# Interleaving the attention of token thirds 2 and 3 with the layers, and a regrouped seven-product scheme with results kept in four PSUM banks

## The chip, the cores and the metric

The kernel runs on one core of a Trainium2 chip. The metric is the device time of one execution in microseconds (us); the median of repeated executions counts. A profile of one execution gives the engines' timelines: TensorE (PE, with its weight loads PEld), VectorE (DVE), ScalarE (ACT), GpSimd (POOL) and the queue of SyncE (SP) that issues the transfers.

## What is computed

Windowed attention, then a gated layer, then a second gated layer whose last two matrices stand one behind the other. All is fp32.

```python
# q, k, v: (4, 8, 576, 64); window 128; ALiBi slopes by head
scores = q @ k.T / sqrt(64) + bias            # masked to 0 <= rel < 128
attn = softmax(scores) @ v
x = attn.transpose(0, 2, 1, 3).reshape(2304, 512)
x = (sigmoid(x @ w_gate) * (x @ w_val)) @ w_out          # d_ff 1536
out = ((x @ w1) * (x @ w2)) @ w3 @ w_out2                # d_ff 1024
```

## The kernel before

Every fp32 operand of a product is split into two fp32r parts, hi (a rounded copy, made on ACT) and lo (the rest, a subtraction on DVE or POOL). One product is then three matmuls: hi*hi, hi*lo, lo*hi (function `product`, lines 424 to 426).

**Attention stage.** 16 pairs (batch, two heads) of 5 steps give 80 steps, NSTEP. A software pipeline of 90 slots (SLOTS) runs them, each engine with its own order written out by hand and with lags between the parts: `scores` on PE (for both heads at once, q laid out in blocks on the diagonal over 128 partitions, for up to two query blocks of 64, 256 key columns each), `score` on DVE (bias and row minimum), `exponentials` on ACT, `reciprocals` on DVE, `normalise` on POOL, `turn` on PE (up to four transposes), `turned_hi` on ACT, `turned_lo` on DVE, `pv` on PE, `out_copy` on ACT. Into the same slots go the splits of q, k and v, and 64 products `fold(k)`, which multiply w3 by the last matrix once, so that the second layer needs one matrix less. The activations xf of all 2304 tokens are complete before the layers begin.

**Layer stage.** Tokens go in three passes (NPASS) of 768. In a pass, 6 groups (G1) of 256 hidden columns of layer 1 and 4 groups (G2) of layer 2 follow each other, 30 groups in all. A group has two halves, gate (m=0) and value (m=1). Each half is one 2x2 block multiplication done with seven products of the Strassen kind, `multiply(g, m, ...)`, 42 matmuls of 384 columns, into three banks quad_ps; ACT copies two of them out (`keep_21`, `keep_12`), DVE forms the four results in SBUF (`combine`), ACT applies the gate (Sigmoid in layer 1, Copy in layer 2), DVE multiplies and splits. `project(g)` then makes 8 output tiles of 6 matmuls in three banks o_ps, which DVE adds into xf (`add_up`, 551 ns each). PE runs `project(g-1)` behind the halves of g; after the last group of a layer (`last_of`) its own projection follows at once, and the next layer, an "instance", can start only from its sums: five sums of x blocks on DVE and POOL (`x_sum`), seven hi copies on ACT (`xs_hi_part`), seven lo parts (`x_lo_part`). The order of the products is M2, M4, M5, M3, M1, M7, M6. POOL forms five sums of weight blocks for each half (`weight_sum`) and their lo parts (`weights_lo`). SP loads one half's weights (512 KB) when the ones before have been split.

Of the kernel before, what the change touches and what calls it, by code (L numbers as in the profile page):

```python
# [7 lines left out]
ALU = mybir.AluOpType  # L8
# [4 lines left out]
P = 128  # L13
B, H, S, D = 4, 8, 576, 64
WINDOW = 128
# [3 lines left out]
QB = 64  # L19
NQ = S // QB  # L20
KW = WINDOW + QB
HP = H // 2
PAIRS = B * HP
STEPS = (NQ + 1) // 2
NSTEP = PAIRS * STEPS
VC = (S + P - 1) // P
# [11 lines left out]
NQUAD = 2 * NG  # L38
SCALE = 1.0 / D ** 0.5
MASKED = -1e9  # L40
RAWS = 4


M2, M4, M5, M3, M1, M7, M6 = range(7)

W_S5, W_S2, W_D6, W_D7, W_S1, W_11, W_22 = range(7)
W_OF = {M2: W_S2, M4: W_22, M5: W_S5, M3: W_11, M1: W_S1, M7: W_D7, M6: W_D6}

BANK_OF = {M2: 0, M4: 1, M5: 2, M3: 0, M1: 2, M7: 1, M6: 2}

C11, C12, C21, C22 = 0, 1, 2, 3

HI_IN = {r + 2: r for r in range(IB)}
LO_IN = {r + 3: r for r in range(IB)}

LAG_QK, LAG_SCORE, LAG_NORM, LAG_TURN, LAG_PV, LAG_OUT = 4, 5, 6, 7, 9, 9
LAG_FOLD = 6
NFOLD = IB * IB
SLOTS = NSTEP + LAG_OUT + 1

X_SUM_SLOT = {M4: 48, M3: 54, M1: 60, M7: 66, M6: 72}
X_HI_SLOT = {M2: 48, M4: 49, M5: 52, M3: 55, M1: 61, M7: 67, M6: 73}
X_LO_SLOT = {M2: 50, M4: 51, M5: 53, M3: 57, M1: 63, M7: 68, M6: 75}
W_SUM_SLOT = {71: (0, 0), 72: (0, 1), 73: (0, 2), 77: (1, 0), 78: (1, 1), 79: (1, 2)}
W_HI_SLOT = {74: 0, 80: 1}
W_LO_SLOT = {75: 0, 81: 1}

RAW_SLOT = 66
# [22 lines left out]

def build(nc, qT, kT, v, bias8, ident, w3t, wo2, w_gate, w_val, w_out, w1, w2, outT):
    scratch = nc.dram_tensor("w3_times_wout", (IB, P, DM), F32, kind="Internal").ap()
    ctx = ExitStack()
    with ctx:
        def sb(scope, name, shape, dt):
            return scope.enter_context(nc.sbuf_tensor(name, shape, dt))

        def sem(name):
            return ctx.enter_context(nc.semaphore(name))  # L100

        xf = sb(ctx, "xf", [P, KB * T], F32)
        xs_hi = sb(ctx, "xs_hi", [P, 7 * 2 * TH], F32R)
        xs_lo = sb(ctx, "xs_lo", [P, 7 * 2 * TH], F32R)
        xsum = [sb(ctx, "xsum0", [P, 2 * TH], F32)]

        with ExitStack() as one:
            wo2_raw = sb(one, "wo2_raw", [P, RAWS * DM], F32)
            w3_raw = sb(one, "w3_raw", [P, IB * P], F32)
            w3_hi = sb(one, "w3_hi", [P, IB * P], F32R)  # L110
            w3_lo = sb(one, "w3_lo", [P, IB * P], F32R)
            wo2_hi = sb(one, "wo2_hi", [P, IB * DM], F32R)
            wo2_lo = sb(one, "wo2_lo", [P, IB * DM], F32R)
            q_raw = sb(one, "q_raw", [P, S], F32)
            k_raw = sb(one, "k_raw", [P, S], F32)
            v_raw = sb(one, "v_raw", [P, VC * P], F32)
            q_hi = [sb(one, f"q_hi{b}", [P, NQ * P], F32R) for b in range(2)]
            q_lo = [sb(one, f"q_lo{b}", [P, NQ * P], F32R) for b in range(2)]
            k_hi = [sb(one, f"k_hi{b}", [P, S], F32R) for b in range(2)]
            k_lo = [sb(one, f"k_lo{b}", [P, S], F32R) for b in range(2)]  # L120
            v_hi = [sb(one, f"v_hi{b}", [P, VC * P], F32R) for b in range(2)]
            v_lo = [sb(one, f"v_lo{b}", [P, VC * P], F32R) for b in range(2)]
            bias = sb(one, "bias", [P, HP * KW], F32)
            eye = sb(one, "eye", [P, P], F32)
            negs = [sb(one, f"negs{b}", [P, 2 * KW], F32) for b in range(2)]
            exps = [sb(one, f"exps{b}", [P, 2 * KW], F32) for b in range(2)]
            prob = [sb(one, f"prob{b}", [P, 2 * (2 * P + QB)], F32) for b in range(2)]
            pt_hi = [sb(one, f"pt_hi{b}", [P, 4 * P], F32R) for b in range(2)]
            pt_lo = [sb(one, f"pt_lo{b}", [P, 4 * P], F32R) for b in range(2)]
            negmax = sb(one, "negmax", [P, 4], F32)  # L130
            rowsum = sb(one, "rowsum", [P, 4], F32)
            rowsum2 = sb(one, "rowsum2", [P, 4], F32)
            recip = sb(one, "recip", [P, 4], F32)
            fold_sb = sb(one, "fold_sb", [P, DM], F32)

            pA = [one.enter_context(nc.psum_tensor(f"score_ps{b}", [P, 512], F32)) for b in range(2)]
            fold_ps = [one.enter_context(nc.psum_tensor(f"fold_ps{b}", [P, 512], F32)) for b in range(2)]
            pB = [one.enter_context(nc.psum_tensor(f"turn_ps{b}", [P, 512], F32)) for b in range(2)]
            pC = [one.enter_context(nc.psum_tensor(f"pv_ps{b}", [P, 512], F32)) for b in range(2)]

        raw_q = [sb(ctx, f"raw_q{m}", [P, PIECE], F32) for m in range(2)]
        raw_o = sb(ctx, "raw_o", [P, PIECE], F32)
        wsum = [sb(ctx, f"wsum{m}", [P, 5 * GW], F32) for m in range(2)]
# [3 lines left out]
        wo_hi = [sb(ctx, f"wo_hi{b}", [P, PIECE], F32R) for b in range(2)]  # L147
        wo_lo = [sb(ctx, f"wo_lo{b}", [P, PIECE], F32R) for b in range(2)]
        side = sb(ctx, "side", [P, 4 * TH], F32)
        hid = sb(ctx, "hid", [P, 4 * TH], F32)  # L150
        h_hi = [sb(ctx, f"h_hi{b}", [P, 4 * TH], F32R) for b in range(2)]
        h_lo = [sb(ctx, f"h_lo{b}", [P, 4 * TH], F32R) for b in range(2)]
        s21 = sb(ctx, "s21", [P, TH], F32)
        s12 = sb(ctx, "s12", [P, TH], F32)
        u11 = sb(ctx, "u11", [P, TH], F32)
        t22 = sb(ctx, "t22", [P, TH], F32)
        xsum += [sb(ctx, f"xsum{k}", [P, 2 * TH], F32) for k in range(1, 5)]

        qc = ctx.enter_context(nc.psum_tensor("quad_ps2", [P, 512], F32))
        gate_ps = [ctx.enter_context(nc.psum_tensor("gate_ps0", [P, 512], F32))]  # L160
        qa, qb = [ctx.enter_context(nc.psum_tensor(f"quad_ps{k}", [P, 512], F32)) for k in (0, 1)]
        quad_ps = [qa, qb, qc]
        gate_ps.append(ctx.enter_context(nc.psum_tensor("gate_ps1", [P, 512], F32)))
        ps_o = [ctx.enter_context(nc.psum_tensor(f"o_ps{o}", [P, 512], F32)) for o in range(3)]

        q_in, k_in, v_in = sem("q_in"), sem("k_in"), sem("v_in")
        bias_in, eye_in = sem("bias_in"), sem("eye_in")
        w3_in = [sem("w3_in0"), sem("w3_in1")]
        wo2_in = [sem(f"wo2_in{r}") for r in range(RAWS)]
        small_zeroed = sem("small_zeroed")  # L170
        zeroed = [sem("zeroed_q0"), sem("zeroed_rest")]
        q_hi_done, q_split = sem("q_hi_done"), [sem("q_split0"), sem("q_split1")]
        k_hi_done, k_split = sem("k_hi_done"), sem("k_split")
        v_hi_done, v_split = sem("v_hi_done"), sem("v_split")
        w3_hi_done, w3_split = sem("w3_hi_done"), sem("w3_split")
# [7 lines left out]
        rawq_in, rawo_in = [sem("rawq_in0"), sem("rawq_in1")], sem("rawo_in")  # L183
        wsum_done = [sem("wsum_done0"), sem("wsum_done1")]
        wq_hi_done = [sem("wq_hi_done0"), sem("wq_hi_done1")]
        wq_split = [sem("wq_split0"), sem("wq_split1")]
        wo_hi_done, wo_split = sem("wo_hi_done"), sem("wo_split")
        xsum_done = [sem(f"xsum_done{j}") for j in range(7)]
# [3 lines left out]
        s21_done, s12_done, u11_done = sem("s21_done"), sem("s12_done"), sem("u11_done")  # L192
        t22_done = sem("t22_done")
        c_done = [sem(f"c{k}_done") for k in ("11", "12", "21", "22")]
# [4 lines left out]
        def where(n):  # L199

            return n // STEPS, n % STEPS

        def blocks_of(i):

            return (0, 1) if 2 * i + 1 < NQ else (0,)

        def chunks_of(i):

            return (1,) if i == 0 else (0, 1)

        def seen(i, j):

            return max(0, 2 - (2 * i + j)) * QB

        def two(ap):

            return ap[:, :].rearrange("p (j c) -> p j c", j=2)[:, :, 0:KW]

        def diagonal(x, h):

            return x[h * D:(h + 1) * D, :].rearrange("p (j h c) -> p j h c", h=2, c=QB)[:, :, h, :]

        def blocks(x, h):

            return x[h * D:(h + 1) * D, :].rearrange("p (j c) -> p j c", c=QB)

        def raw_block(r):
            return wo2_raw[:, (r % RAWS) * DM:(r % RAWS + 1) * DM]

        def turned_cols(i):  # L230

            lo, n = chunks_of(i)[0], len(blocks_of(i))
            return lambda ap: ap[:, :].rearrange("p (c n) -> p c n", c=2)[:, lo:2, 0:n * P]

# [915 lines left out]
```

## Time and profile before

| | us |
|---|---|
| median of 3 runs | 971.6 (970.73 to 973.06) |
| the profiled execution's own time | 972.31 |
| its span, first to last instruction | 970.5 |
| PE busy | 899.5 |
| POOL busy | 722.3 |
| DVE busy | 689.1 |
| ACT busy | 505.8 |
| mean granted clock of TensorE | 0.979 |

The span is what the profiler saw of the execution; 1.8 us lie around it. Busy time counts an instruction from its start to its modelled end, and matmuls in a row overlap: a matmul that is recorded with 0.33 us starts 0.17 us behind the one before it. For PE, the distance from start to start is the price, not the recorded duration.

### The profile page before, as it was taken

The numbers are of one execution on the slowest core, as the hardware profiler recorded it, in microseconds if no ns is written. First come the engines' busy times: TensorE is split into PE (matmuls) and PEld (weight loads), VectorE is DVE, ScalarE is ACT, GpSimd is POOL, SyncE is SP. The second block draws the span as 40 slices with busy tenths as digits, with TensorE's granted clock in tenths as the row PEclk, the third lists the DMA queues.
The fourth block names the chain that finished last, engine by engine and source line by source line (L and its number), as shares of the span: only waits on it lengthen the run. The fifth ranks groups of instructions, "written<-read, shape, count | busy, mean of one in ns | idle before, by whom it ended". The sixth has DMA issues, their size and how long they took to land.

```text
span 970.5 us, 15723 instructions
## 1 busy us (share of the span) xinstructions
PE 899.5 (93%) x5272; PEld 869.0 (90%) x5272; DVE 689.1 (71%) x1506; ACT 505.8 (52%) x1139; POOL 722.3 (74%) x535
## 2 busy tenths in 40 slices
PE   3999989868999997999999999799999999989998
PEld 3889877767899997899889999789988999988998
DVE  7988899885666668577756666857785666686666
ACT  4888878767544443544454444354444444435441
POOL 6778877876887775998679777489867977738940
PEclk9999999979999999999999999999999999998999
DMA  7333432410222210222142222012113211211301
GB/s 235 105 108 113 121 95 78 143 47 23 86 76 78 66 66 22 72 82 69 41 140 79 66 83 71 22 66 87 66 44 131 87 66 66 67 42 52 102 1 66
DMA packets 37409, 75.92 MB, mean 78 GB/s; under 512 B 3153, under 2 KB 16081, under 8 KB 37329
## 3 DMA queue, kind: packets, MB, share of 16 engines
q1 hardware_dynamic: 37328, 74.92, 23.9%
q8 instruction: 42, 0.69, 0.3%
q14 instruction: 39, 0.31, 0.1%
HBM read 68.09 MB, written 6.82 MB: 77 GB/s over the span
## 4 chain that ended last, share of the span: by engine, by line
PE 71%; DVE 14%; ACT 7%; issue 5%; POOL 2%; DMA 1%; SPq 0%; ACTq 0%; DVEq 0%; POOLq 0%
PE quad_ps L424 15%; PE quad_ps L426 14%; PE quad_ps L425 14%; PE o_ps L424 8%; PE o_ps L426 8%; PE o_ps L425 8%; DVE rowsum L766 3%; DVE xs_lo L811 2%; ACT exps L584 2%; DVE negs L755 1%; DVE xf L879 1%; POOL prob L1007 1%; ACT pt_hi L595 1%; DVE pt_lo L775 1%; ACT wq_hi L630 1%
## 5 line engine op out<-in xcount | busy, mean ns | idle before, releaser
L424 PE MATMUL quad_ps<-xs_hi,wq_hi 128*128 128x384 f32 x840 | 286.9, 342 | 25.4 <-ACT s L646 22.0
L426 PE MATMUL quad_ps<-xs_hi,wq_lo 128*128 128x384 f32 x840 | 284.6, 339 | 0.0
L425 PE MATMUL quad_ps<-xs_lo,wq_hi 128*128 128x384 f32 x840 | 284.5, 339 | 0.0
L424 PEld LDWEIGHTS quad_ps<-xs_hi,wq_hi 128*128 128x128 f32 x840 | 160.8, 191 | 31.7 <-issue 16.5
L1041 POOL TENSOR_TENSOR wq_lo<-wsum,wq_hi 128x1280 fp32r<-128x1280 f32 x60 | 177.3, 2955 | 9.4 <-ACT wq_hi L630 9.4
L424 PE MATMUL o_ps<-h_hi,wo_hi 128*128 128x384 f32 x480 | 161.2, 336 | 3.2 <-DVE xf L879 3.1
L425 PEld LDWEIGHTS quad_ps<-xs_lo,wq_hi 128*128 128x128 f32 x840 | 160.7, 191 | 0.0
L426 PEld LDWEIGHTS quad_ps<-xs_hi,wq_lo 128*128 128x128 f32 x840 | 160.5, 191 | 0.0
L426 PE MATMUL o_ps<-h_hi,wo_lo 128*128 128x384 f32 x480 | 160.4, 334 | 0.0
L425 PE MATMUL o_ps<-h_lo,wo_hi 128*128 128x384 f32 x480 | 160.4, 334 | 0.0
L1037 POOL TENSOR_TENSOR wq_lo<-raw_q,wq_hi 128x512 fp32r<-128x512 f32 x60 | 77.7, 1295 | 105.8 <-ACT wq_hi L624 105.8
L879 DVE TENSOR_TENSOR xf<-o_ps,xf 128x384 f32<-128x384 f32 x192 | 103.5, 551 | 43.6 <-PE o_ps L426 43.6
L661 ACT ACTIVATE gate_ps<-side 128x384 f32<-128x384 f32 x120 | 59.6, 498 | 76.4 <-DVE h_lo L867 55.4
L424 PEld LDWEIGHTS o_ps<-h_hi,wo_hi 128*128 128x128 f32 x480 | 90.1, 188 | 5.8 <-DVE xf L879 5.8
L646 ACT COPY s<-quad_ps 128x384 f32<-128x384 f32 x60 | 28.7, 479 | 120.2 <-PE quad_ps L426 120.1
L425 PEld LDWEIGHTS o_ps<-h_lo,wo_hi 128*128 128x128 f32 x480 | 90.1, 188 | 0.0
L426 PEld LDWEIGHTS o_ps<-h_hi,wo_lo 128*128 128x128 f32 x480 | 90.1, 188 | 0.0
L668 ACT CAST h_hi<-gate_ps 128x384 fp32r<-128x384 f32 x120 | 57.6, 480 | 59.6 <-DVE gate_ps L862 59.6
L1047 POOL TENSOR_TENSOR wo_lo<-raw_o,wo_hi 128x1024 fp32r<-128x1024 f32 x30 | 72.0, 2401 | 17.9 <-ACT wo_hi L638 17.9
L584 ACT ACTIVATE exps<-negs,negmax 128x192 f32<-128x192 f32 (+1 forms) x144 | 62.0, 432 | 42.9 <-DVE negmax L755 40.9
L867 DVE TENSOR_TENSOR h_lo<-gate_ps,h_hi 128x384 fp32r<-128x384 f32 x120 | 65.9, 549 | 23.8 <-ACT h_hi L668 23.3
L1062 POOL TENSOR_TENSOR wsum<-raw_q 128x512 f32<-128x512 f32 x60 | 81.8, 1363 | 0.0
(89 smaller groups left out, 1893.8 us busy)
## 6 DMA issues: line engine op xcount, KB each, us to landing
raw_q<-w SPq DMA_DIRECT2D x24, 512.0 KB, 3.5
raw_q<-w_gate SPq DMA_DIRECT2D x18, 512.0 KB, 3.5
raw_q<-w_val SPq DMA_DIRECT2D x18, 512.0 KB, 3.5
raw_o<-w_out SPq DMA_DIRECT2D x18, 512.0 KB, 3.5
raw_o<-w_times_wout SPq DMA_DIRECT2D x12, 512.0 KB, 3.6
k_raw<-kT SPq DMA_DIRECT2D x16, 288.0 KB, 2.9
q_raw<-qT SPq DMA_DIRECT2D x16, 288.0 KB, 3.0
v_raw<-v SPq DMA_DIRECT2D x16, 256.0 KB, 2.7
```

The lines of the kernel that those rows point to most:

```text
L424: pe.matmul(out, lh, rh, start=start, stop=False, skip_group_check=onto)
L425: pe.matmul(out, lh, rl, start=False, stop=False, skip_group_check=onto)
L426: return pe.matmul(out, ll, rh, start=False, stop=stop, skip_group_check=onto)
L584: op = nc.scalar.activation(exps[buf][:, cols], negs[buf][:, cols], ACT.Exp, scale=-1.0, bias=negmax[:, 2 * buf + j:2 * buf + j + 1], accu ...
L661: nc.scalar.activation(gate_ps[n % 2][:, 0:TH], side[:, piece(k)], func).then_inc(gated, 1)
L668: nc.scalar.copy(h_hi[g % 2][:, piece(k)], gate_ps[n % 2][:, 0:TH]).then_inc(h_hi_done, 1)
L867: nc.vector.tensor_tensor(out=h_lo[g % 2][:, piece(k)], in0=gate_ps[n % 2][:, 0:TH], in1=h_hi[g % 2][:, piece(k)], op=ALU.subtract).then_i ...
L879: op = nc.vector.tensor_tensor(out=xf[:, cols], in0=ps_o[t % 3][:, 0:TH], in1=xf[:, cols], op=ALU.add)
L1037: nc.gpsimd.tensor_tensor(out=wq_lo[m][:, cols].rearrange("p (b n) -> p b n", b=2), in0=four[:, 0:4:3, :], in1=wq_hi[m][:, cols].rearrange ...
L1041: nc.gpsimd.tensor_tensor(out=wq_lo[m][:, 0:5 * GW], in0=wsum[m][:, :], in1=wq_hi[m][:, 0:5 * GW], op=ALU.subtract).then_inc(wq_split[m], 1)
L1047: nc.gpsimd.tensor_tensor(out=wo_lo[g % 2][:, :], in0=raw_o[:, :], in1=wo_hi[g % 2][:, :], op=ALU.subtract).then_inc(wo_split, 1)
L1062: op = nc.gpsimd.tensor_tensor(out=out[:, 2 * GW:4 * GW], in0=raw[:, 0:2 * GW], in1=raw[:, 2 * GW:4 * GW], op=ALU.subtract)
```

## The change

The number of attention steps stays 80, but they are cut by token third: a job is (third, pair of heads, batch, first query, steps), a step has 128 queries of two heads. The first third (28 steps) runs ahead of the layers, in 36 slots together with all 64 folds, two to a slot; the 24 steps of the second third run inside pass 0 of the layers, and the 28 of the third inside pass 1, one in each "section" (a half or a projection; 30 sections in a pass). Scores are multiplied for each head by itself, 64 contraction rows, into a bank of each head. The small addition to the row sum moves from DVE to ACT. The layers use another form of the seven products: four operand sums in place of five for x and for the weights, products P2 and P4 accumulated onto P1 and P7 in PSUM, the results left in their four banks, where gate, product and split read them. One bank copy a half on ACT (`keep`) and five additions on DVE stand in place of two copies and six additions. The projection has two banks in place of three, since two banks are now attention's. xf holds two thirds of the tokens' columns in place of three.

```diff
+PARTS = (((0, 0, 3), (0, 384, 2), (1, 0, 2)), ((1, 192, 3), (2, 0, 3)), ((2, 384, 2), (3, 0, 3), (3, 384, 2)))
+JOBS = [(third, hp, b, q0, n) for third in range(NPASS) for hp in range(HP) for b, q0, n in PARTS[third]]
...
-BANK_OF = {M2: 0, M4: 1, M5: 2, M3: 0, M1: 2, M7: 1, M6: 2}
+BANK_OF = {P1: 0, P2: 0, P6: 1, P3: 1, P5: 2, P7: 3, P4: 3}
+BANK_OUT = {C11: 0, C12: 1, C22: 2, C21: 3}
...
-LAG_QK, LAG_SCORE, LAG_NORM, LAG_TURN, LAG_PV, LAG_OUT = 4, 5, 6, 7, 9, 9
+LAG_QK, LAG_SCORE, LAG_NORM, LAG_TURN, LAG_PV = 3, 4, 5, 6, 8
+SLOTS = HEAD + LAG_PV
...
+def fold_slot(k):
+
+    return 5 + k // 2
...
+        quad = [ps(f"quad_ps{k}") for k in range(4)]
+        ps_o = [ps(f"o_ps{k}") for k in range(2)]
+        attn = [ps(f"attn_ps{k}") for k in range(2)]
...
+            sp.wait_ge(zeroed, 1)
+            load_k(0)
...
+                sides = ((q_hi, k_hi), (q_hi, k_lo), (q_lo, k_hi))
+                for t, (left, right) in enumerate(sides):
+                    for h in range(2):
+                        rows = slice(h * D, (h + 1) * D)
+                        mm = pe.matmul(score_bank(n, h)[:, keys], left[st][rows, q], right[st][rows, where],
+                                       start=t == 0, stop=t == 2)
+                mm.then_inc(qk_done, 1)
...
+            for sec, (g, kind, of) in enumerate(SECTIONS):
+                n, m = step_at(sec), step_at(sec - 1)
+                if n is not None:
+                    scores(n)
+                if kind == "proj":
+                    for k in range(8):
+                        project(of, k)
+                        if k == 1 and m is not None:
+                            turn(m)
+                        if k == 5 and m is not None:
+                            pv(m)
+                else:
+                    for j in range(7):
+                        multiply(2 * g + (kind == "val"), j)
+                        if j == P5 and m is not None:
+                            turn(m)
+                        if j == P7 and m is not None:
+                            pv(m)
...
+            def keep(q):
+
+                act.wait_ge(prod_done, product_done(q, P1))
+                wait(act, u2_done, q)
+                nc.scalar.copy(s1[:, :], quad[0][:, 0:TH]).then_inc(s1_done, 1)
...
+            def sums_26(q):
+
+                dve.wait_ge(prod_done, product_done(q, P6))
+                dve.wait_ge(s1_done, q + 1)
+                wait(dve, c_done[C21], q)
+                nc.vector.tensor_tensor(out=u2[:, :], in0=quad[1][:, 0:TH], in1=s1[:, :], op=ALU.add
+                                        ).then_inc(u2_done, 1)
+                dve.wait_ge(u2_done, q + 1)
+                wait(dve, c_done[C12], q)
+                nc.vector.tensor_tensor(out=u25[:, :], in0=quad[2][:, 0:TH], in1=u2[:, :], op=ALU.add
+                                        ).then_inc(u25_done, 1)
...
+                elif kind == "val":
+                    sums_26(2 * g + 1)
+                    if m is not None:
+                        turned_lo(m)
+                    if n is not None:
+                        reciprocals(n)
+                    hidden(g, C11)
+                    result_22(2 * g + 1)
+                    hidden_lo(g, C11)
+                    hidden(g, C22)
+                    result_12(2 * g + 1)
+                    hidden(g, C12)
+                    hidden_lo(g, C22)
+                    result_21(2 * g + 1)
...
+                elif g % GP == G1 - 1:
+                    for k in range(3):
+                        add_up(of, k)
+                    if m is not None:
+                        turned_lo(m)
+                    if n is not None:
+                        reciprocals(n)
+                    add_up(of, 3)
+                    x_sum(inst, P5)
+                    add_up(of, 4)
+                    add_up(of, 5)
+                    x_sum(inst, P6)
+                    x_lo(inst, P5)
```

The products of a half run in the order P1, P5, P6, P2, P7, P3, P4; P2 waits for `keep`, P3 for the sum u2, P4 for result C22 in its bank. The first product into each bank waits for the gate (on a value half) or for the lo split (on a gate half) that reads the bank last.

## Rows read from the trace of the kernel before

**Rows 1.** The page: span, and the share of each engine's busy time.
```profile
span 970.5 us, 15723 instructions
PE 899.5 (93%) x5272; PEld 869.0 (90%) x5272; DVE 689.1 (71%) x1506; ACT 505.8 (52%) x1139; POOL 722.3 (74%) x535
```
**Rows 2.** Busy time by stretch: PE, PEld, DVE, ACT, POOL, clock, DMA.
```profile
60.00:90.00 30.00, 29.14 (x206) 26.14 (x204) 26.74 (x97) 25.24 (x88) 24.03 (x28) 1.00 0.40 114
...
238.00:968.00 730.00, 700.98 (x3947) 691.82 (x3946) 490.48 (x885) 323.52 (x544) 539.79 (x332) 0.98 0.20 68
...
256.00:370.00 114.00, 114.00 (x656) 113.68 (x657) 72.16 (x142) 49.17 (x84) 88.35 (x56) 1.00 0.22 74
...
370.00:403.00 33.00, 26.51 (x141) 25.58 (x140) 26.09 (x37) 16.63 (x26) 22.62 (x14) 0.95 0.10 34
469.00:508.00 39.00, 35.20 (x187) 33.27 (x186) 24.90 (x41) 15.48 (x27) 27.76 (x18) 0.96 0.28 94
```
**Rows 3.** PE in order of time, layer stage: start, us; 65 starts apart.
```profile
405.58 0.33 PE L425 MATMUL quad_ps<-xs_lo,wq_hi 128*128 128x384 f32 x1
...
416.85 0.33 PE L424 MATMUL o_ps<-h_hi,wo_hi 128*128 128x384 f32 x1
```
**Rows 4.** PE in order of time where an instance begins.
```profile
384.17 0.45 PE L424 MATMUL quad_ps<-xs_hi,wq_hi 128*128 128x384 f32 x1 [4.95 <-ACT s L646]
384.42 0.52 PE L425 MATMUL quad_ps<-xs_lo,wq_hi 128*128 128x384 f32 x1
...
387.89 0.34 PE L424 MATMUL quad_ps<-xs_hi,wq_hi 128*128 128x384 f32 x1
```
**Rows 5.** Who waited for whom: total us, times, longest.
```profile
PE quad_ps L424 <- ACT s L646: 22.0, 8, 4.9
```
**Rows 6.** PE in order of time, one attention slot and its fold.
```profile
63.30 0.28 PE L425 MATMUL score_ps<-k_lo,q_hi 128*128 128x256 f32 x1
...
63.89 0.28 PE L424 MATMUL pv_ps<-pt_hi,v_hi 128*128 128x256 f32 x1
...
64.26 0.60 PE L455 MATMUL turn_ps<-eye,prob 128*128 128x128 f32 x4
64.61 0.48 PE L424 MATMUL fold_ps<-wo_hi,w_hi 128*128 128x512 f32 x1
...
65.16 0.40 PE L426 MATMUL fold_ps<-wo_hi,w_lo 128*128 128x512 f32 x1
```
**Rows 7.** Groups by line and shape: busy us, mean ns, idle before.
```profile
L1041 POOL TENSOR_TENSOR wq_lo<-wsum,wq_hi 128x1280 fp32r<-128x1280 f32 x60 | 177.3, 2955 | 9.4 <-ACT wq_hi L630 9.4
L1047 POOL TENSOR_TENSOR wo_lo<-raw_o,wo_hi 128x1024 fp32r<-128x1024 f32 x30 | 72.0, 2401 | 17.9 <-ACT wo_hi L638 17.9
L1065 POOL TENSOR_TENSOR wsum<-raw_q 128x256 f32<-128x256 f32 x60 | 48.7, 812 | 0.0
L584 ACT ACTIVATE exps<-negs,negmax 128x192 f32<-128x192 f32 x112 | 50.3, 450 | 37.0 <-DVE negmax L755 36.3
L755 DVE CUSTOM_DVE_ANT_0 negs<-score_ps,bias 128x192 f32<-128x192 f32 x112 | 34.9, 343 | 0.0
L775 DVE TENSOR_TENSOR pt_lo<-turn_ps,pt_hi 128x512 fp32r<-128x512 f32 x48 | 33.0, 688 | 3.9 <-ACT pt_hi L595 3.6
```
**Rows 8.** ACT in order of time at the first Sigmoid.
```profile
239.69 0.48 ACT L652 COPY s<-quad_ps 128x384 f32<-128x384 f32 x1
240.19 1.28 ACT L661 ACT_TABLE_LOAD   x1
241.49 0.49 ACT L661 ACTIVATE gate_ps<-side 128x384 f32<-128x384 f32 x1
```
**Rows 9.** Start and end: first load, first fold, last addition.
```profile
0.73 0.39 SPq L313 DMA_DIRECT2D k_raw<-kT  x1
...
17.00 0.63 PE L424 MATMUL fold_ps<-wo_hi,w_hi 128*128 128x512 f32 x1
...
967.65 0.56 DVE xf L879
```

More of the change, by code:

```diff
@@ L119, in build @@
[L119 to L126, printed above, removed]
@@ L1025, in x_lo_part, with x_sum @@
-            def x_lo_part(inst, j):
+                cols = heads(soft[buf])[0:rows, :, keys]
+                nc.gpsimd.tensor_tensor(
+                    out=cols, in0=cols,
+                    in1=recip[0:rows, 2 * buf:2 * buf + 2].unsqueeze(2).to_broadcast([rows, 2, keys.stop - keys.start]),
+                    op=ALU.mult).then_inc(norm_done, 1)
+            def x_sum(inst):
+                wait_x(pool, inst, P7)
+                wait(pool, xs_split[P7], inst)
+                nc.gpsimd.tensor_tensor(out=pair_of(xt[2][:, :]), in0=b_block(inst, 1, 1), in1=b_block(inst, 0, 1),
+                                        op=ALU.subtract).then_inc(t_done[P7], 1)
@@ new lines, in _ @@
+                if s == 30:
+                    plain_lo(0, 0)
+                    sums_lo(0, 0)
+                if s == 32:
+                    weight_sums(0, 1)
+                if s == 34:
+                    plain_lo(0, 1)
+            x_sum(0)
+            for j in (P7, P3, P4):
+                x_lo(0, j)
+            for sec, (g, kind, of) in enumerate(SECTIONS):
+                n = step_at(sec)
+                more, inst = g + 1 < NG, instance(g) + 1
+                if kind == "gate":
+                    sums_lo(g, 1)
+                    if more:
+                        weight_sums(g + 1, 0)
+                elif kind == "val":
+                    out_lo(g)
+                    if more:
+                        weight_sums(g + 1, 1)
+                elif of == g - 1 and more:
+                    plain_lo(g + 1, 0)
+                    sums_lo(g + 1, 0)
+                if n is not None:
+                    normalise(n)
+                splits(sec)
+                if kind == "val" and first_of(g):
+                    plain_lo(g + 1, 0)
+                    sums_lo(g + 1, 0)
+                    plain_lo(g + 1, 1)
+                if kind == "proj" and of == g - 1 and more:
+                    plain_lo(g + 1, 1)
+                    if g % GP == GP - 1:
+                        x_lo(inst, P1)
+                if kind == "proj" and of == g and more:
+                    if g % GP == G1 - 1:
+                        x_lo(inst, P1)
+                    x_sum(inst)
+                    for j in (P7, P3, P4):
+                        x_lo(inst, j)
```

1497 lines of the change are left out of this document (775 added, 722 removed).

## The prediction

> **What bounds the kernel now.** The page comes first: PE is busy for 93% of the span, POOL for 74% [rows 1]. A mean over stages says little, so I read busy time by stretch next [rows 2]. In the attention stretch from 60 to 90 us PE has 29.1 of 30 us, DVE 26.7, ACT 25.2, POOL 24.0: all four are close to full, and none of them can be relieved alone. In the steady layer stretch from 256 to 370 us PE has all of it, POOL 78%, DVE 63%, ACT 43%. So the layers have free time on three engines, and attention has none on any. The third view is PE in order of time. In steady layers 65 starts lie within 11.27 us, 0.1733 us for a matmul of 384 columns [rows 3]. From 238 to 968 us there are 3947 matmuls, 684 us at that rate out of 730 [rows 2]: 46 us are lost. The losses sit where an instance begins: from 370 to 403 us 141 matmuls (24.4 us of work) take 33 us, 8.6 us lost, three times in the kernel; from 469 to 508 us 187 (32.4) take 39, 6.6 us lost, twice. PE there waited 4.95 us for the first bank copy, itself late behind seven x splits, and then ran for some 3.5 us at half the rate, 0.315 us a matmul, so at the lower level of its clock, 1.2 GHz [rows 4]. Such waits sum to 22.0 us over the kernel [rows 5].
>
> The time before is, in these terms: 235 us until the layers alone hold PE (two products are already among the last attention steps), 3960 x 0.1733 = 686 us, 46 us lost and 3 us behind the last matmul (the last addition starts at 967.65 [rows 9]). That is 970 us, and the execution has 1.8 us around its span, 972.3; the median is 0.7 us lower.
>
> **The head: what is left ahead of the layers.** A full attention step costs PE: six score matmuls (63.30 to 63.89 is five of them, 0.12 each) 0.71 us, six of pv 0.73, four transposes 0.35 (64.26 to 64.61) [rows 6]: 1.8 us. The start of a batch saves about 0.9 of it (128 keys, one chunk); 8 of the first 28 steps are such. A fold is three matmuls of 512 columns, two starts in 0.55 us and a third near 0.22, some 0.73 us [rows 6]; two in a slot make 1.45. Mean slot on PE: 1.8 - 0.26 + 1.45 = 3.0 us. DVE: score twice, 343 ns at 192 columns [rows 7], so about 0.93 at 256 with the reads of the minimum, the lo part 0.69, the reciprocal 0.17, and the splits of v and w3 and the copies of the fold about 1.0: 2.8. POOL: normalise about 1.1, k, q and v lo 1.3, w3 0.4: 2.8. ACT 2.5. In the stretch of rows 2 PE kept 97% with DVE at 89%, so a slot takes 3.1 us. The first fold stands at 17.0 us [rows 9]. The change holds SP back until DVE has cleared six tiles (about 2.4 us), with the first load at 0.73 before, but it asks for fewer bytes by the first step and waits for no buffer: 19 us. Then 28 slots x 3.1 = 87, three slots with little in them 5, and the last eight folds 5.8, which cover the x sums of POOL and DVE. **Head: 117 us** (bounds 108 and 130: all slots at PE's 3.0 with the old start, and 3.5).
>
> **The layers.** Products and projections keep their number: 3960 x 0.1733 = **686 us**. The 52 moved steps now cost PE time that nothing covers: 52 x 1.8 - 8 x 0.9 = **86 us**. This is the price of the move; 118 us of head go against it.
>
> **Losses at instances.** The form with four sums needs x only by tiles: P1 wants two output tiles, P5 four, and the first bank copy stands ahead of nothing that is late. I follow the end of layer 1: with the last tile done at T, P1 starts at T, P5 at T+1, P6 waits for x_sum, hi and lo on DVE until T+3.2 (1.1 late), P4 0.7 late. With no long pause there is nothing that lowers the clock. 2 us three times, 1 us twice; the second group, which follows with no projection between, waits for lo splits of the value half, 1.5 us six times: **17 us** in place of 46 (bounds 8 and 46).
>
> **Losses inside sections.** Here the trace of before shows nothing like it. The short loop is turn, hi on ACT, lo on DVE, pv: about 1.6 us with handovers, against three products of 1.04 us between turn and pv, but DVE has to make u2 and u25 first, and these wait for P6: the lo part is ready 3.05 us after the turn, pv comes at 3.12. The other orders have 1 us or more to spare: P4 waits for C22 with pv and P3 between. So most sections fit and some miss by tenths; I take 0.3 us, 52 x 0.3 = **16 us** (bounds 0, and 1.5 us a step, a late engine in each section, near the longest DVE piece between two duties). Per group of 28 us POOL has: eight block sums of 812 ns, 6.5; lo of 768 and 1024 columns for two halves, about 8.5 (between 812 ns at 256 and 2955 at 1280); wo_lo 2.4 [rows 7]; normalise 2.6 to 3.0; q, k, v lo 2.9 to 4.9. That is 23 to 25 us, under PE, with slack of a section between each product of POOL and its use. DVE has 26 operations of about 0.5 us and 5 us of attention, 19; DMA is at a fifth [rows 2]. DVE's last value operation runs 1.6 us into the projection, which the two banks just bear.
>
> **The table of ACT.** Exp and Sigmoid did not share a table: at the first Sigmoid a load of 1.28 us stands, and the activation begins 0.02 us behind it [rows 8]. In passes 0 and 1 the 12 groups of layer 1 alternate twice each, 24 loads, 31 us of ACT. ACT then has about 21 of 28 us in such a group, and the gate it delays is wanted 2 us later: nothing on the path. It costs 0.5 us each if the value half's lo part falls behind it, which is in my upper bound.
> The Trainium skill (ScalarE: Activation LUTs, "What ACT_TABLE_LOAD costs") adds a drain of about 1.38 us to each switch, 64 us of ACT in place of 31; the row shows no such gap. By the page ACT would be near 24 of 28 us, and the sum for PE would move to its upper bound.
>
> **Sum.** 117 + 686 + 86 + 17 + 16 + 3 = 925 us of span, 926.8 with what lies around it, some 0.7 less as a median: **926 us**, 4.7% below 971.6. A measurement of this kernel can tell 0.2%, 2 us, from no change.
>
> **Rivals.**
> *The two heads overlap on PE.* Each head's scores use 64 rows and a bank of their own, interleaved. If pairs run together, six matmuls cost three: 0.35 us less, 52 times in the layers, 18 us, and nothing in the head, where DVE and POOL are as full: 908 us. No row here has a matmul of 64 rows, so the trace speaks neither way.
> The Trainium skill states such overlap (TensorEngine Tiling (Array Packing), "Theoretical Speedup", up to 2x) and that a change of tiling mode drains PE ("Key Properties"); two drains a step would give back part of the gain, and no row shows either.
> *The losses at instances stay.* If x splits still gate the first half (POOL's lo part of 768 columns lasts about 2 us), the 17 us go back to 46: 955 us. Against it: P1 and P5 no longer wait for seven splits.
> *A late lo part in each section.* At 0.8 us a step, 26 us more: 952 us.
> *Slower than before.* One mechanism: the fixed orders of DVE and ACT chain turn, lo and pv behind a product's sums each time, and PE stands in all 52 steps. It decides at 0.3 + 45/52 = 1.2 us a step. At 1.5 us: 926 + 62 = 988 us. For it: DVE's margin in the loop is under 0.1 us and table loads lengthen ACT's part. Against it: one miss can't be longer than the operation ahead.
>
> **Chances.** Forecast, 915 to 940 us: 0.50. Heads overlap, 898 to 915: 0.20. Instances or lo parts, 940 to 962: 0.16. Slower: 0.10. Else, under 898 or near 971: 0.04. Range 898 to 962 leaves 0.14 out. Faster by over 0.2%: 0.87; within: 0.02; slower: 0.11.
>
> **What would show it.** In the changed kernel's PE timeline: the first product of the layers near 117 us; score matmuls at 0.12 us from start to start (0.06 for the overlap); no pause over 2 us at instance starts and no stretch at 0.32 us a matmul; waits of pv for the lo part under 0.3 us in the mean; 25 table loads or so on ACT. A head over 130 us, or waits of PE for DVE beyond 30 us in sum, would make it wrong.

## The result, and the profile after

The changed kernel takes 1018.9 us (median of 4 runs, 1016.8 to 1020.5), the kernel before 972.0 beside it: ratio 1.0482 (1.0457 to 1.0506), 4.8% slower. The forecast was 926, its range 898 to 962. Both its size and its sign were wrong. Two of the experiments below, e10 and e12, had one execution each that was far slower than its fellows (4918 and 1744 us); it is left out of their times.

The page of the changed kernel, answering to [rows 1]:

```profile
span 1017.9 us, 16149 instructions
PE 919.8 (90%) x5352; PEld 855.0 (84%) x5352; DVE 602.1 (59%) x1364; ACT 549.9 (54%) x1259; POOL 737.3 (72%) x626
```

Busy time by stretch (the stretch, its length, then PE, PEld, DVE, ACT, POOL, clock, DMA share, GB/s). First the head in three stretches, then the six stretches in which an instance begins, then the whole layer stage; the second block has the five between the starts:

```profile
19.00:60.00 41.00, 37.79 (x226) 28.13 (x224) 25.38 (x86) 25.99 (x93) 25.91 (x29) 1.00 0.34 107
60.00:110.00 50.00, 44.34 (x272) 33.51 (x269) 31.55 (x104) 34.13 (x122) 35.69 (x42) 0.97 0.43 137
110.00:134.00 24.00, 18.63 (x95) 14.60 (x94) 14.39 (x28) 13.14 (x35) 21.30 (x21) 0.93 0.12 39
134.00:168.00 34.00, 27.84 (x158) 26.00 (x157) 17.68 (x41) 22.95 (x46) 32.50 (x26) 0.90 0.38 132
310.00:352.00 42.00, 30.70 (x173) 28.73 (x172) 26.55 (x48) 22.19 (x48) 37.30 (x25) 0.88 0.12 39
425.00:470.00 45.00, 33.24 (x179) 30.76 (x178) 24.69 (x50) 21.47 (x42) 33.52 (x27) 0.90 0.27 90
620.00:662.00 42.00, 30.08 (x166) 27.94 (x165) 26.74 (x48) 21.33 (x48) 33.83 (x26) 0.88 0.13 42
745.00:780.00 35.00, 24.70 (x125) 23.24 (x124) 17.11 (x23) 12.21 (x18) 23.59 (x17) 0.90 0.25 91
900.00:945.00 45.00, 35.83 (x183) 34.28 (x182) 27.03 (x38) 18.28 (x29) 34.86 (x26) 0.92 0.18 60
134.00:1015.00 881.00, 816.10 (x4754) 776.47 (x4752) 521.84 (x1125) 467.53 (x990) 647.49 (x525) 0.97 0.22 72
```
```profile
168.00:310.00 142.00, 140.50 (x866) 131.85 (x865) 86.27 (x217) 94.08 (x215) 105.74 (x89) 1.00 0.25 81
352.00:425.00 73.00, 72.91 (x437) 70.82 (x436) 44.37 (x97) 37.83 (x79) 55.20 (x47) 1.00 0.19 63
470.00:620.00 150.00, 148.69 (x906) 138.93 (x905) 86.97 (x222) 99.73 (x235) 112.06 (x103) 1.00 0.26 84
662.00:745.00 83.00, 82.56 (x506) 77.82 (x505) 49.29 (x121) 48.05 (x121) 63.18 (x58) 1.00 0.19 64
780.00:900.00 120.00, 119.78 (x682) 117.92 (x681) 72.97 (x142) 49.07 (x81) 86.47 (x67) 1.00 0.21 71
```

In the five stretches between, PE has 564.4 of 568 us at a granted clock of 1.00. The steady sections run as they were meant to, with the moved steps inside. The six stretches of the starts last 243 us, hold 984 starts of PE, and the clock there is 0.88 to 0.92. If every one of them were a full matmul of 384 columns at 0.1733 us, they would fill 171 us, so at least 72 us are lost there (attention's matmuls are shorter). POOL is the busiest engine in four of the six (37.3 of 42 us, 32.5 of 34).

Against the sum, whose head and layer stage were 117 and 805 us: the layers begin at 134 (the head is 17 us too long), and the layer stage lasts 881, which is 686 + 86 + 109 of losses where 33 were forecast.

One start is that from pass 0 to pass 1. Its chain, in three views in order of time (start, duration), is SP's queue, then ACT, then PE:

```profile
440.90 0.40 SPq L501 DMA_DIRECT2D outT<-xf  x1
441.34 0.50 SPq L479 DMA_DIRECT2D raw_q<-w_gate  x1
441.89 1.02 SPq L488 DMA_DIRECT2D wo_lo_raw<-w_out  x1
```
```profile
450.03 1.04 ACT L818 CAST wo_hi<-wo_lo_raw 128x1024 fp32r<-128x1024 f32 x1 [6.61 <-DMA wo_lo_raw<-w_out]
451.09 1.28 ACT L837 ACT_TABLE_LOAD   x1
452.38 0.49 ACT L837 ACTIVATE sig<-quad_ps 128x384 f32<-128x384 f32 x1
```
```profile
453.02 0.66 PE L576 MATMUL quad_ps<-xs_hi,wq_hi 128*128 128x384 f32 x1 [4.65 <-ACT sig L837]
...
454.11 0.52 PE L576 MATMUL quad_ps<-xs_hi,wq_hi 128*128 128x384 f32 x1
...
455.07 0.52 PE L576 MATMUL quad_ps<-xs_hi,wq_hi 128*128 128x384 f32 x1
...
467.77 0.69 PE L576 MATMUL quad_ps<-xs_hi,wq_hi 128*128 128x384 f32 x1 [3.62 <-POOL wq_lo L1290]
```

The store of a finished pass (1.57 MB) stands ahead of the next loads in SP's queue; `w_out` lands some 8 us after its issue (typical: 3.5). ACT waits for it 6.61 us to split it, and behind that split stand a table load and the gate that frees the bank PE wants: a pause of 4.65 us. Then PE runs three starts in 0.96 us, 0.32 each, where 0.17 is usual: the lower level of its clock (1.2 GHz), until about 457. Some fifteen microseconds after the first pause it pauses again, now for POOL's lo part of the weight sums.

The other kind of start, layer 1 to layer 2 in pass 0, on DVE and PE:

```profile
322.81 1.93 DVE L1013 TENSOR_TENSOR xs_lo<-xf,xs_hi 128x768 fp32r<-128x768 f32 x1 [3.41 <-ACT xs_hi L804]
324.67 2.55 DVE L1007 TENSOR_TENSOR xt<-xf,xt 128x768 f32<-128x768 f32 x1
327.14 0.41 DVE L954 CUSTOM_DVE_ANT_0 soft<-attn_ps,bias 128x256 f32<-128x256 f32 x1
```
```profile
328.05 1.09 PE L614 MATMUL attn_ps<-eye,soft 128*128 128x128 f32 x4 [7.03 <-DVE negmax L954]
```

PE stands for 7.03 us ahead of `turn`. It writes into an attention bank that still holds the next step's scores, and `score`, which reads them, is queued on DVE behind an x split and an x sum. I had named no such wait: the turn of one step waits for the score of the next.

### The profile page after: what moved, and what is told of

It reads as the page before. It is cut to its first block, busy times and chain, and to the rows that moved or that the text cites. A ratio compares the mean times of both kernels' runs of the same rounds, so it can differ in the third digit from the quotient of the medians.

```text
span 1017.9 us, 16149 instructions
## 1 busy us (share of the span) xinstructions
PE 919.8 (90%) x5352; PEld 855.0 (84%) x5352; DVE 602.1 (59%) x1364; ACT 549.9 (54%) x1259; POOL 737.3 (72%) x626
## 4 chain that ended last, share of the span: by engine, by line
PE 71%; POOL 13%; DVE 7%; issue 4%; DMA 2%; ACT 1%; SPq 1%; DVEq 0%; POOLq 0%; ACTq 0%
PE quad_ps L576 13%; PE quad_ps L578 12%; PE quad_ps L577 12%; PE o_ps L576 8%; PE o_ps L578 7%; PE o_ps L577 7%; POOL wq_lo L1290 2%; PE attn_ps L599 2%; PE attn_ps L576 2%; PE attn_ps L614 2%; POOL xs_lo L1254 2%; DMA wo_lo_raw<-w_out 2%; POOL wq_lo L1283 1%; POOL soft L1239 1%; DVE xf L1072 1%
## 5 line engine op out<-in xcount | busy, mean ns | idle before, releaser
L576 PE MATMUL quad_ps<-xs_hi,wq_hi 128*128 128x384 f32 x840 | 296.8, 353 | 36.4 <-POOL wq_lo L1290 17.8
L576 PE MATMUL o_ps<-h_hi,wo_hi 128*128 128x384 f32 x480 | 167.0, 348 | 10.5 <-DVE xf L1072 10.0
L1021 DVE TENSOR_TENSOR u<-quad_ps,s 128x384 f32<-128x384 f32 x60 | 33.5, 558 | 196.6 <-PE quad_ps L578 195.2
L1290 POOL TENSOR_TENSOR wq_lo<-wsum,wq_hi 128x1024 fp32r<-128x1024 f32 x60 | 143.5, 2392 | 7.7
L1239 POOL TENSOR_TENSOR soft<-soft,recip 128x512 f32<-128x512 f32 (+2 forms) x80 | 73.4, 918 | 96.0 <-DVE recip L965 95.8
L1283 POOL TENSOR_TENSOR wq_lo<-raw_q,wq_hi 128x768 fp32r<-128x768 f32 x60 | 110.6, 1843 | 36.4 <-ACT wq_hi L810 36.4
L771 ACT ACTIVATE soft<-soft,negmax 128x256 f32<-128x256 f32 (+2 forms) x160 | 75.0, 470 | 52.3 <-DVE negmax L954 52.2
L843 ACT CAST h_hi<-quad_ps 128x384 fp32r<-128x384 f32 x120 | 57.3, 478 | 83.2 <-DVE quad_ps L1055 82.6
L1296 POOL TENSOR_TENSOR wo_lo<-wo_lo_raw,wo_hi 128x1024 fp32r<-128x1024 f32 x30 | 71.8, 2394 | 19.6 <-ACT wo_hi L818 19.6
L837 ACT ACTIVATE sig<-quad_ps 128x384 f32<-128x384 f32 x120 | 58.1, 491 | 39.3 <-DVE quad_ps L1044 14.9
```

The costliest lines, as they stand in the source:

```text
L576: pe.matmul(out, lh, rh, start=start, stop=False, skip_group_check=onto)
L771: op = nc.scalar.activation(cols, cols, ACT.Exp, scale=-1.0, bias=negmax[0:rows, 2 * buf + h:2 * buf + h + 1], accum_out=rowsum[0:rows, 2 ...
L837: nc.scalar.activation(sig[:, piece(blk)], quad[BANK_OUT[blk]][:, 0:TH], func).then_inc(gated, 1)
L843: nc.scalar.copy(h_hi[g % 2][:, piece(blk)], quad[BANK_OUT[blk]][:, 0:TH]).then_inc(h_hi_done, 1)
L1021: nc.vector.tensor_tensor(out=u2[:, :], in0=quad[1][:, 0:TH], in1=s1[:, :], op=ALU.add).then_inc(u2_done, 1)
L1239: nc.gpsimd.tensor_tensor(out=cols, in0=cols, in1=recip[0:rows, 2 * buf:2 * buf + 2].unsqueeze(2).to_broadcast([rows, 2, keys.stop - keys. ...
```

## The experiments

Fifteen kernels ran. Each time is a median, taken beside the kernel before (971.5 to 972.7 us); "saves" and "costs" are against the changed kernel's 1018.9. Where medians differ by 2 or 3 us, the runs do not tell them apart.

| | edit | us | ratio to before (95%) |
|---|---|---|---|
| e1 | store behind the next loads | 1009.3 | 1.0384 (1.0366 to 1.0403) |
| e2 | POOL: weight lo parts first | 1023.6 | 1.0520 (1.0482 to 1.0558) |
| e3 | x splits in another order | 1027.4 | 1.0552 (1.0517 to 1.0586) |
| e4 | e1, e2 and e3 | 1008.3 | 1.0367 (1.0336 to 1.0398) |
| e5 | no moved steps | 903.7 | 0.9292 (0.9267 to 0.9316) |
| e6 | the two heads' scores one after the other | 1020.1 | 1.0492 (1.0471 to 1.0512) |
| e7 | Exp as the gate | 1016.9 | 1.0454 (1.0427 to 1.0481) |
| e8 | all lo parts of w3 on DVE | 1008.8 | 1.0375 (1.0358 to 1.0391) |
| e9 | one lo part off POOL in first groups | 1020.0 | 1.0502 (1.0483 to 1.0522) |
| e10 | POOL: added work in first groups | 1034.0 | 1.0649 (1.0622 to 1.0676) |
| e11 | POOL: the same in steady groups | 1017.8 | 1.0484 (1.0458 to 1.0509) |
| e12 | e4, e8 and e9 | 995.6 | 1.0242 (1.0216 to 1.0268) |
| e13 | e5, e4 and e8 | 886.1 | 0.9118 (0.9093 to 0.9143) |
| e14 | e1, e3, e8; x lo part of P1 first | 1000.6 | 1.0296 (1.0279 to 1.0312) |
| e15 | e12; x lo part of P1 first | 993.4 | 1.0222 (1.0197 to 1.0247) |

**The moved steps alone (e5).** The 52 steps are left out with their loads and splits, and thirds 2 and 3 of x are a constant or old columns.

```diff
 def step_at(sec):
-    return n if t < NPASS and n < STEPS_TO[t + 1] else None
+    return None
```

> The 52 attention steps of thirds 2 and 3, their loads and splits are left out (the layers then work on a constant and on old columns in their place); the first third, the folds and all layer work stay. Theory of the moved steps' price: PE work 52 x 1.65, 86 us, sections 16 us, and some 35 us that POOL loses at the instance starts where it has their normalise and splits as well: 137 us less than the changed kernel, about 882 us. Rival (the instance losses belong to the new form of the seven products and to its x splits, not to attention): only the 102 us go, about 917 us, with waits at the instance starts as long as now.

903.7 lies between my 882 and the rival's 917. The steps cost 115.2 us, 2.2 each, against 102 forecast (86 of PE and 16 inside sections). So the larger part of the miss is there without them. From 134 us to the end of its span at 901 are 767 us; less 685 of products (3951 starts) and 3 of tail, 79 are lost with no attention in the layers at all, against 46 before. Its windows, a start, the steady stretch behind it, and the layer change:

```profile
134.00:166.00 32.00, 25.30 (x134) 24.06 (x133) 14.24 (x25) 15.72 (x26) 31.47 (x25) 0.95 0.30 107
166.00:272.00 106.00, 106.00 (x606) 104.75 (x605) 64.41 (x125) 40.54 (x67) 72.82 (x56) 1.00 0.20 65
272.00:312.00 40.00, 31.07 (x154) 29.51 (x153) 24.67 (x34) 15.92 (x24) 30.01 (x21) 0.87 0.17 55
```

The steady 106 us hold 606 starts, 105 us of work: nothing is lost. The first start loses 32 - 23.2 = 8.8, the layer change 40 - 26.7 = 13.3. The loss is the starts'. POOL is busy for 31.5 of 32 us in the first. What PE waited for in the layers of e5 (total us, times, longest):

```profile
PE quad_ps L581 <- POOL wq_lo L1295: 12.6, 6, 4.2
PE quad_ps L581 <- ACT s L829: 10.4, 3, 3.5
PE quad_ps L581 <- ACT sig L842: 9.9, 3, 4.1
PE o_ps L581 <- DVE xf L1077: 7.8, 7, 1.9
PE quad_ps L581 <- DVE xs_lo L1018: 6.8, 7, 1.5
```

These are 47.5 us; before, such waits of the layers were 28.3. In stretches behind the pauses some 106 starts come 0.32 us apart, about 16 us more. The second row is the wait for the first bank copy [rows 5], come back at each layer change; the copy stands on ACT behind the hi copy for P4, whose x sum DVE makes last:

```profile
287.81 0.94 DVE L1012 TENSOR_TENSOR xt<-xf,xt 128x768 f32<-128x768 f32 x1
288.86 0.83 ACT L809 CAST xs_hi<-xt 128x768 fp32r<-128x768 f32 x1 [3.80 <-DVE xt L1012]
289.60 0.47 ACT L829 COPY s<-quad_ps 128x384 f32<-128x384 f32 x1
290.22 0.66 PE L581 MATMUL quad_ps<-xs_hi,wq_hi 128*128 128x384 f32 x1 [3.46 <-ACT s L829]
```

**The store (e1).** It moves from ahead of the gate half's load to behind the value half's.

```diff
-                    if g and g % GP == 0:
-                        store_pass(g // GP - 1)
...
+                if kind == "val" and g and g % GP == 0:
+                    store_pass(g // GP - 1)
```

> Theory (each instance start loses time to one order of its own): the store of a finished pass, 1.57 MB, goes into SP's queue behind the second half's weights instead of ahead of the first half's. In the changed kernel the matrix w_out landed 8 us after its issue, ACT stood 6.6 us in front of it with the gate behind it, and PE waited 4.7 and 5.2 us at the two pass starts and then ran some 4 us at 0.32 us a matmul. Expected: both waits under 1 us, 10 to 13 us less in all, about 1007 us. Rival (the moved attention steps themselves overload ACT and DVE, and the stall only moves to the next wait): under 4 us less.

1009.3, 9.6 us saved at two pass starts. In the trace PE's waits for the gate fall from 10.6 to 0.6 us. Shown.

**Orders at the start (e2, e3, e4).** e2 makes POOL split the next half's weights ahead of its normalise and attention splits. e3 puts the lo part of P2 and the x sum of P4 on DVE behind the score, and the hi copy for P4 on ACT behind `keep`. The first lines are e2's, the others e3's.

```diff
+                if kind == "val" and first_of(g):
+                    plain_lo(g + 1, 0)
+                    sums_lo(g + 1, 0)
...
+                    if g % GP == G1:
+                        x_lo(instance(g), P2)
+                        x_sum(instance(g), P4)
```

> Theory: in the value half of an instance's first group POOL makes the lo parts of the next group's first half ahead of normalise and of the k and q splits, since no projection stands before that group. PE waited 2.4 to 4.7 us for these parts at four places where attention steps run. Expected: these waits shorter by 1.5 to 3 us each, with the half-rate stretch behind them, 8 to 14 us less, about 1007 us. Rival: POOL is simply full there (12 us of work in a 9 us section), so that the order changes nothing and turn waits for normalise instead: within 3 us of the changed kernel.

> Theory: at the change from layer 1 to layer 2 the last x sum and the lo part of P2 on DVE go behind the attention step's score, the hi part of P4 on ACT goes behind the first bank copy, and the hi part of P2 goes ahead of P7's. In the changed kernel the transposes stood 7.0 and 5.7 us until DVE had made that score (in passes 0 and 1), and in pass 2 P2 stood 3.5 us for the bank copy. Expected: 10 to 18 us less over three places, about 1004 us. Rival (the seven splits are the bound there whatever their order): under 4 us less, with the waits named after an x split.

> The three orders together. Theory (independent losses): the sum of the single gains, 28 to 45 us less than the changed kernel, 975 to 990 us, with PE's loss in the six instance starts down from about 88 to about 50 us. Rival (one common limit, the moved steps): the gains overlap and the sum stays under half of that, above 1000 us.

e2 and e3 each shorten the wait they aim at, and both are slower, by 4.7 and 8.5 us, which neither theory nor rival foresaw. e4 takes no more than the store's gain, as its rival said. The waits of PE (total us, times, longest), the changed kernel first, then e3, whose profiled execution was its fastest (1020.9) and so does not show all of the 8.5:

```profile
PE quad_ps L576 <- POOL wq_lo L1290: 17.8, 5, 4.6
PE attn_ps L614 <- DVE negmax L954: 12.7, 2, 7.0
```
```profile
PE quad_ps L576 <- POOL wq_lo L1293: 23.0, 7, 4.9
```

The turn's wait has fallen to 1.3 us, and that for POOL's weights has grown by 5.2. e2 shortens that same wait to 7.6 us, and PE waits at the scores instead: there its waits rise from 3.4 to 12.1 us, 4.3 of them for k's lo part; for the longest, 3.8 us, the profile names no other engine.

**POOL at the start (e10, e11).** One block sum of weights is made four times over, in the value half that prepares the gate of the second group (six times in the kernel). In e11 the condition is `g % GP in (4, 9)`: as often, in steady groups.

```diff
+                for _ in range(3 if m == 1 and g > 0 and first_of(g - 1) else 0):
+                    nc.gpsimd.tensor_tensor(out=out(W_S1), in0=blk(A21), in1=blk(A22), op=ALU.add
+                                            ).then_inc(again, 1)
```

> POOL makes one weight sum (0.74 us) four times in place of once in the value half of each instance's first group, six times 2.2 us and three handovers more. Theory (POOL bounds there): the whole dose comes out, 13 us and what the clock adds, 13 to 20 us more, about 1035 us. Rival (slack is left on POOL): under 4 us more.

> The same dose in six other groups, inside a layer (the value halves of groups 3 and 8 of each pass), the control of the run before. Theory: POOL has a section of slack there even beside attention steps, no change within 3 us, 1017 to 1021 us. Rival (POOL is at its limit in all of passes 0 and 1, 23 to 25 of 28 us a group): 8 us more or above.

The same work costs 15.1 us at the starts, 2.5 a time, and nothing (-1.1) elsewhere. A sum lasts 0.74 us there, so three are 2.2 us plus handovers: what POOL gets more at a start, PE waits for in full. In e10's trace the wait for POOL's weight lo parts rises from 17.8 to 25.9 us.

**Relief of POOL at the start (e9).** In first groups DVE makes the lo part of the output weights (2.4 us on POOL).

> In the first group of each instance the lo part of w_out (2.4 us on POOL) is made on DVE behind its last work of the value half. Theory (POOL is the bound from the x splits of an instance to the start of its second group, so stalls taken away elsewhere came back as waits for its wq_lo): each of six waits for wq_lo shorter by up to 2.4 us, 8 to 16 us less, about 1007 us. Rival (DVE and the handovers bound there, not POOL): within 3 us, or slower by DVE's 1.3 us each.

1020.0, no gain, a miss for my theory and a hit for the rival: added load costs all of itself, removed load brings nothing. The wait for POOL falls from 17.8 to 13.8 us, but PE now stands up to 1.2 us for DVE's lo parts of the hidden values, and the mean clock is 0.965, 0.971 in the changed kernel. That DVE too has no room there is what this suggests; no dose on DVE was tried.

**The head (e8).** The lo parts of w3 that POOL made go to DVE.

```diff
-                if s in W3_LO_SLOT and W3_LO_SLOT[s] % 2:
+                if s in W3_LO_SLOT:
```

> In the head all 16 lo halves of w3 are made on DVE (1.0 us each) and none on POOL (1.3 us each). In the changed kernel PE stood 11 us for POOL's at seven folds. Theory (POOL's order, normalise and splits ahead of these, sets the slots): 8 to 12 us less, about 1008 us, head of 124 in place of 134 us. Rival (PE and DVE are full in the head as forecast): within 3 us.

1008.8, 10.1 us saved. Its first product of the layers starts at 122.57 us in place of 134.80:

```profile
122.57 0.44 PE L575 MATMUL quad_ps<-xs_hi,wq_hi 128*128 128x384 f32 x1
```

**Heads and table (e6, e7).** e6 swaps the loops over heads and terms; e7 computes Exp in place of Sigmoid, another function, so that the table is never switched.

> The same score matmuls, but three of one head behind each other and then three of the other, so that neighbours use the same 64 rows. Theory (pairs of the two heads do run together now, six starts in 0.56 us, and the change of mode costs what that gains): without the pairs a step's scores take 0.36 us more, in the layers 52 x 0.36, 19 us more, about 1037 us. Rival (no overlap, the trace only shows starts together): no change, within 4 us.

> The gate of layer 1 uses Exp in place of Sigmoid (another function is computed), which takes away 24 table loads of 1.28 us on ACT. Theory (they lie beside PE's work save at first groups): 2 to 8 us less. Rival (the fixed order of ACT carries each load to PE, 1.3 us each): 25 to 31 us less.

Neither matters beyond the noise: 1020.1 and 1016.9. A set of scores in the changed kernel, with the matmul before and behind it:

```profile
207.74 0.34 PE L578 MATMUL quad_ps<-xs_hi,wq_lo 128*128 128x384 f32 x1
208.00 0.39 PE L599 MATMUL attn_ps<-k_hi,q_hi 64*128 64x256 f32 x2
208.23 0.28 PE L599 MATMUL attn_ps<-k_lo,q_hi 64*128 64x256 f32 x2
208.34 0.29 PE L599 MATMUL attn_ps<-k_hi,q_lo 64*128 64x256 f32 x2
208.56 0.44 PE L576 MATMUL o_ps<-h_hi,wo_hi 128*128 128x384 f32 x1
```

Each row is two matmuls (x2) that start together, so the heads do overlap, in e6 just as well. But 208.00 comes 0.26 us behind the matmul before, not 0.17, and the first pair holds 0.23, not 0.11. From 207.74 + 0.17 to 208.56 it is 0.65 us, and the matmul behind is late by another 0.1: 0.75, as much as the 0.71 forecast without overlap. So it is in all 29 such sets without a wait (median 0.75), while six matmuls of 128 rows and 256 columns, those of pv, take 0.74 with 0.01 us at either end. The rival was right on the overlap and wrong on its worth: it is eaten at the change between shapes. No run has scores that do not overlap; e6 changes the order alone. The Trainium skill says that a change of tiling mode drains PE (TensorEngine Tiling (Array Packing), "Key Properties"); the trace agrees, with about 0.1 us on either side here, though the matmul behind the transposes, which keep 128 rows, is late by 0.09 too.

**Together (e12, e13, e14, e15).** e14 adds POOL's x lo part for P1 ahead of the normalise.

```diff
+                if kind == "proj" and of == g and more and g % GP == G1 - 1:
+                    x_lo(inst, P1)
...
-                    if g % GP == G1 - 1:
-                        x_lo(inst, P1)
```

> The three orders, w3's lo halves on DVE and the first groups' w_out lo part on DVE, together. Theory (POOL's load at the instance starts is the common limit of the three orders, so that taking load from it lets them count): 1008 of the three orders, 10 less in the head, 10 to 16 less from the relief and some of the order's own gain: 978 to 988 us. Rival (still bound by the moved steps): above 995 us.

> As the run without the 52 moved steps (903.7 us), with the three orders and w3's lo halves on DVE. Theory (the orders cost their stalls by themselves, and with the moved steps the gain is eaten by POOL, which has their normalise and splits as well): head 10 us, store 10 us, x order and lo parts 10 us or more: 868 to 876 us. Rival (the x splits of the new form bound there whatever the order): only head and store pay, above 882 us.

> Store later, x order, w3's lo halves on DVE, and at the end of layer 1 POOL makes the lo part of P1 ahead of the step's normalise and of the k and q splits. Theory (this queue holds P1 by 1.9 us and all x splits behind it at two places): 3 to 8 us below a version without it (about 1000), 992 to 997 us. Rival (turn then waits for normalise by as much): 998 us or above.

> All edits together: three orders, w3's lo halves and the first groups' w_out lo part on DVE, P1's lo part first. Theory: the best of them, 986 to 994 us, still slower than the kernel before by about 2%, since the steps' 2.2 us each in the layers (115 us) and the remaining instance losses stand against 101 us less ahead of the layers. Rival (orders interlock): equal to the version without P1's order, 996 us.

With all edits the kernel takes 993.4 us, the best form found, still 2.2% slower than before. 25.5 us are gained; e1 and e8 alone account for 19.7. In e12, e13 and e14 the rival came true, in e15 the theory. e14 has neither e9's relief nor e2's order and stands at 1000.6, 7.2 us above e15; alone the two cost 1.1 and 4.7, and no run tells which of them pays here. e13 is without the steps: 17.5 us below e5, no more than the 19.7 of store and head, so the orders bring nothing there either. Its wait for the first bank copy falls from 10.4 to 1.8 us, and that for POOL's weights, 12.6 in e5, doubles:

```profile
PE quad_ps L580 <- POOL wq_lo L1297: 25.5, 9, 4.9
```

e15's waits of PE:

```profile
PE o_ps L575 <- DVE xf L1075: 10.7, 12, 2.8
PE attn_ps L598 <- issue: 10.6, 6, 5.9
...
PE attn_ps L575 <- DVE pt_lo L975: 7.1, 3, 3.6
PE quad_ps L575 <- POOL wq_lo L1302: 6.8, 4, 3.2
```

The wait for weights has shrunk from 17.8 to 6.8 us, and part of the time has gone to waits for the projection's additions, at the scores and for lo parts of attention: the starts stay full.

## Why the prediction was wrong

In forecast terms: 926 + 17 (head) + 62 (layers without the steps: 79 lost in place of 17) + 13 (steps) = 1018. In terms of before: the head falls by 101 us (235 to 134), the moved steps cost 115, and the layers without them lose about 33 more than they did (79 for 46). 972 - 101 + 115 + 33 = 1019. (The 79 is e5's, counted from 134 us; its first product of the layers starts at 132.16, so some 2 us of the steps' price lie in the head.)

**The price of the move** was right within 13 us: 115 for 102. Some 10 of these are work that the 1.8 us left out. By the medians of the changed kernel's trace a full step holds PE for 0.75 us of scores, 0.74 of pv and 0.44 of transposes, 1.94; over the 52 steps, short ones too, an estimate from such medians gives 96 us for 86. PE was the bound in both stages [rows 2], so a step costs it about as much inside the layers (2.2 us) as it did ahead of them. "This is the price of the move; 118 us of head go against it": it left 118 against 102, a profit of 16 us. The larger part of the forecast gain, 29 of 45, hung on the next term.

**Losses at instances** is the step that failed: "17 us in place of 46". The six stretches of the starts in e5 alone have 224 us for 931 matmuls, 161 us of work: 63 lost, and the rest of its 79 lies next to them. I followed only the first half and only two products' inputs. Missing were:
- The x splits, which still gate the first half at a layer change: in e5 PE waits 10.4 us for the first bank copy and 6.8 for x lo parts, 17 us, as much as my term for all losses.
- POOL's load. In the start of 310 to 352 it has the normalise, k and q lo parts, four x lo parts and an x sum, then the weights: it is busy for 37.3 of 42 us. The dose shows that it has no room there (e10 against e11), and e13 that its weights are the longest wait even without attention. e9 shows that it is not the only bound.
- The store ahead of the loads: 9.6 us (e1). "The first bank copy stands ahead of nothing that is late" was about ACT's queue, and there late work stood: at a pass start a split waiting for a load ahead of the gate, at a layer change a hi copy ahead of the bank copy. I never walked SP's queue past the pass.
- The turn's wait for the next step's score, through a shared bank: 7.0 us at its longest, 12.7 in two.
- "With no long pause there is nothing that lowers the clock". Pauses of up to 7.0 us came, and behind the one at 453 PE ran 12 matmuls at 1.2 GHz, 4.0 us for 2.1 of work.

So of the rivals "the losses at instances stay" had the right place, the right mechanism for a part (17 of 47.5 us of waits in e5) and too small a price (46; 79 came). "Slower than before" had the right sign and the wrong mechanism: it put 1.5 us on each of 52 sections, and sections lose little. Of 115 us for the steps some 96 are work; 19 over 52 sections is under 0.4 as a bound, a part of it at the starts.

**The head: 117**, measured 134. The first fold came at 17.96 us (forecast 19). The missing is in the slots: 28 x 3.1 was too low. The lo parts of w3 alternate between DVE and POOL, and POOL was the late one, for 10 us (e8; 5 or 6 of the 17 stay unexplained); I had put its slot at 2.8 and PE's at 3.0 and let neither wait for the other. PE is busy for 18.6 of the last 24 us and POOL for 21.3.

**Right, and shown:** the table loads, 25 of 1.28 us, cost about 2 us, within the noise (e7); the matmuls of the layers at 0.173; the heads' overlap adds nothing.

The Trainium skill has it that GpSimd and a DVE instruction with two SBUF inputs take turns at a shared port (SBUF — State Buffer, "Who interferes with whom"). The x sums of DVE, minimum, median and maximum of their durations:

```profile
L1007 DVE TENSOR_TENSOR xt<-xf,xt x12: 942/1080/2550, 129.8 to 915.9; 128x768 f32<-128x768 f32 x12
```

The one at 324.67 took 2.55 us beside a lo part of POOL of 2.51 that began at 323.89: from POOL's end at 326.40 to its own at 327.22 is 0.82, near the shortest of these, so the trace agrees. By this, work taken from POOL and given to DVE would be relief in part only, which would bear on e9. That is argued; no run separates it.

**What stays open.** The store, the head and POOL's want of room are shown. Of the 79 us, 47.5 are waits with a name and some 16 the slow clock behind them; about 16 I can't place. A wait's length is not what its removal brings: store and other edits gained some 15 us at the starts, and no run shows what bounds them in the end. PE waits for the additions from the projection's banks for 7.8 us in e5 and 3.1 before; whether two banks in place of three, or the fused form itself, is the reason was not tried.

## What to carry to other kernels

Moving work out of a full stage into one whose free time is on other engines saves only what those engines do; if the bound engine is the same in both, count the move as zero and see what it adds. At a transition, write every engine's queue out to the second unit of work, transfers and shared banks too, and sum each engine's load over that window: if one is full, reordering moves the wait (e2, e3, e4, e13). An added dose, at the suspected place and at a control place, tells an engine without room from one that is merely busy in two runs; it does not tell that the engine is the only bound (e9).

## What the runs showed of the hardware

- Two matmuls on rows 0 to 63 and 64 to 127 start together whichever order the program lists them in (changed kernel and e6); six of 256 columns take 0.56 us from first start to the next matmul's, and about 0.2 us more around them, in all as much as six of 128 rows (0.74).
- A wait of 4.65 us was followed by 12 matmuls 0.32 us apart, at the lower level of the clock.
- With a store of 1.57 MB ahead of it in one queue a load of 512 KB landed some 8 us after its issue, where 3.5 is typical; with the store behind the loads the wait for it was gone (e1).
